# Fused attention and experts: two heads of a pair in row tiles of 64, and twenty bias blocks moved between the first expert matmuls

## The chip, the core and the metric
The kernel runs as one program on one core of a Trainium2 chip. The metric is the device time of one execution in microseconds; three runs of the kernel before gave 641.36, 644.32 and 647.19 us, median 644.32. All inputs and the output are float32 and lie in DRAM. PE is the matrix engine; DVE is VectorE, ACT is ScalarE, POOL is GpSimd, and SP is the engine whose queue issues nearly all transfers.

## The reference
```python
# attention: B, H, S, D = 2, 8, 576, 64
scores = D**-0.5 * q @ k.T
pos = arange(S)
rel = abs(pos[:, None] - pos[None, :])
x = log1p(rel) / log1p(maximum(pos[:, None], 1))
h = maximum(x[..., None] @ w1 + b1, 0)        # 32 hidden units
bias = h @ w2                                  # one value per head
scores = scores + bias.transpose(2, 0, 1)[None]   # the same for both batches
attn = exp(scores - max(scores, -1))
attn = attn / (sum(attn, -1) + 1e-9)
x = (attn @ v) as rows (B*S, H*D) = (1152, 512)
# experts: E, F = 4, 1024
p = domain_probs / (domain_probs.sum(-1) + 1e-9)
out = sum over e of p[:, e] * (maximum(x @ w1[e], 0) @ w2[e])
```
Every expert works on every row.

## The kernel before, in words
The engines run side by side, each with its own instruction stream, and meet at semaphores. The order of the work is written out by hand for each engine; there is no planner.

**Bias blocks.** The bias of all heads is made once, in 36 blocks of 16 query rows, and written to a DRAM scratch, from where it is read back in rows of 128. A block has four `hidden` tiles of 128 x 576: DVE makes three (L573), ACT one (L745), in a ring of three blocks. PE multiplies each with a weight block of 32 columns (L874), so that four such products fill one score bank (column tiles of 32; the trace records each of these matmuls twice). ACT scales the sums into one of four row buffers (L752), and SP stores them (L395). The two score banks alternate.

**Split into high and low parts.** Score and expert matmuls use the type float32r. A number is split in a rounded high part and the rest, and a product is made of three or four partial products. For q and k POOL does this per head ("unit"): q and k of one head, D = 64 rows, are loaded twice, onto both halves of the 128 partitions; `q_parts` holds q's high part on one half and its low part on the other, and so one matmul over 128 rows against `k_hi`, and one against `k_lo`, give all four partial products (L900). A block of 128 query rows takes four matmuls, two for each half of 288 key columns.

**Attention in two parts.** Rows 0 to 255 of each sequence come first (f = 0), the other 320 later (f = 1). There are 8 pairs of heads. A pair has four blocks of 128 rows in part 0 (two per head), and in part 1 four and a fifth that holds the last 64 rows of both heads. A block goes: score (PE, L900), bias added and maximum found (DVE, L590), exp and row sum (ACT, L770), reciprocal (DVE, L600 and L603), normalised (DVE in part 0, L610; POOL in part 1, L540), transposed (PE, L918 and L922, into the turn banks), copied (ACT L776, DVE L616). Then come the products with v (PE, L940: the two heads side by side as column tiles of 64), and x is split (ACT L782, DVE L622). In part 0 both score banks are used in turn, so the next block's scores are made while a block is read; in part 1 only bank 0 is, and the two halves of bank 1 belong to the experts.

**Experts.** The four experts run first on the 512 early rows (ge 0 to 3, each 16 positions: 8 hidden tiles and 4 output tiles in two halves), then on the other 640 (ge 4 to 7). Weights come in chunks of 512 KB; ACT makes the high part (L796), DVE the low part (L628). A hidden tile is 12 or 24 matmuls (L960), an output tile 24 (L977), in a ring of three banks (`M_RING`). Between the positions of ge 0 to 3 stand the "slots" of attention part 1, six for each pair, from position 0 on; 50 of the 64 positions have one.

`split_count`, `score`, `turn`, `products` and `slot` (PE), `add_bias`, `invert` and `normalise` (DVE), and `load_raw`, `load_bias0`, `load_bias1` and `store_rows` (SP) are the functions that the change rewrites.

Of the kernel before, what the change touches and what calls it, by code (L numbers as in the profile page):

```python
# [9 lines left out]
ALU = mybir.AluOpType  # L10
# [20 lines left out]

TABLE_W = 2 * S - G
# [5 lines left out]
ON_DVE = QUADS - 1  # L38

# [4 lines left out]
UNITS = 2 * PAIRS  # L44
# [3 lines left out]
Q_W = ROWS0 + 3 * D  # L48
TURNS = (5, 7)

# [4 lines left out]
SLOTS = 6  # L55
CHUNK = 1024
# [12 lines left out]
def kq_slot(u):  # L69
    return u % 5 if u < UNITS else (u - UNITS + 1) % 3  # L70


def last_block_of(u):

    f, p, side = u // UNITS, u % UNITS // 2, u % 2
    return blk(0, p, 2 * side + 1) if f == 0 else blk(1, p, 4)


def before_in_slot(u):

    return next((o for o in range(u - 1, -1, -1) if kq_slot(o) == kq_slot(u)), None)


ACT_TURNS = ((0, 1, 3), (0, 1, 2, 3, 4, 5, 6))
# [80 lines left out]
M_RING = 3  # L165


def attention_and_experts(nc, qk_t, v, b_w, probs_in, w1, w2,
# [3 lines left out]
    with ExitStack() as top:  # L172
# [13 lines left out]
        k_hi = sb(top, "k_hi", [P, 3, S], F32R)  # L186
        k_lo = sb(top, "k_lo", [P, 3, S], F32R)
        q_parts = sb(top, "q_parts", [P, 3, Q_W], F32R)
# [3 lines left out]
        probs_t = sb(top, "probs_t", [P, 2, JT, ROWS1])  # L192
        ident = sb(top, "ident", [P, P])
# [13 lines left out]
        with ExitStack() as early:  # L207
            hidden_sb = sb(early, "hidden", [P, HID_RING, QUADS, S])
            rows = sb(early, "rows", [P, ROW_RING, S])
            table = sb(early, "table", [P, TABLE_W])  # L210
            probs_2 = sb(early, "probs_2", [P, BLKS[0], S])
            bias_2 = sb(early, "bias_2", [P, BLKS[0], S])
            kx_hi = sb(early, "kx_hi", [P, 2, S], F32R)
            kx_lo = sb(early, "kx_lo", [P, 2, S], F32R)
            qx_parts = sb(early, "qx_parts", [P, 2, ROWS0], F32R)
# [8 lines left out]
        turn_bank = [top.enter_context(nc.psum_tensor(f"turn{r}", [P, 512], F32)) for r in range(2)]  # L224
# [12 lines left out]
        v_in = [sem(f"v_in{r}") for r in range(4)]  # L237
        bias0_in = [sem(f"bias0_in{r}") for r in range(2)]
        bias1_in = [sem(f"bias1_in{r}") for r in range(3)]
        qk_split, scored, maxed, exped = (sem(s) for s in ("qk_split", "scored", "maxed", "exped"))  # L240
        plus_eps, recip_done, normed0, normed1 = (
            sem(s) for s in ("plus_eps", "recip_done", "normed0", "normed1"))
# [7 lines left out]
        SMALL_DMAS, CLEARED = G + 1, 4  # L250


        def hidden(n, quad):
            return hidden_sb[:, n % HID_RING, quad, :]
# [5 lines left out]
        def k_of(u):  # L260
            s = kq_slot(u)
            return (k_hi[:, s, :], k_lo[:, s, :]) if s < 3 else (kx_hi[:, s - 3, :], kx_lo[:, s - 3, :])

        def q_of(u):
            s = kq_slot(u)
            return q_parts[:, s, :] if s < 3 else qx_parts[:, s - 3, :]

        def split_count(u):

            return 4 * (u + 1) if u < UNITS else 4 * UNITS + 6 * (u + 1 - UNITS)  # L270
# [7 lines left out]
        def score_of(n):  # L278
            return score_bank[n % 2 if n < BLKS[0] * PAIRS else 0]

        def m_bank(n):
            return (score_bank[1][:, 0, :], score_bank[1][:, 1, :], last_bank[:, :])[n % M_RING]

        def sub_in(f, n, i):
            bank = turn_bank[n % 2]
            if i < 4:
                return bank[:, :].rearrange("p (t q) -> p t q", t=4)
            if i == 4:
                return bank[0:J_LAST, :].rearrange("p (r q) -> p r q", r=2)
            if i == 5:  # L290
                return bank[:, :].rearrange("p (t r q) -> p t r q", t=4, r=2)
            return bank[0:J_LAST, 0:P].rearrange("p (r q) -> p r q", r=2)

        def sub_out(f, i):
            if i < 4:
                return probs_t[:, i // 2, 0:4, P * (i % 2):P * (i % 2) + P]
            if i == 4:
                return probs_t[0:J_LAST, :, 4, 0:ROWS0]
            if i == 5:
                return probs_t[:, :, 0:4, ROWS0:ROWS1].rearrange("p r t q -> p t r q")  # L300
            return probs_t[0:J_LAST, :, 4, ROWS0:ROWS1]

        def x_slice(x, f, p):
            m, b = p // 2, p % 2
            first = ROWS0 * b if f == 0 else TOK0 + ROWS1 * b
            return x[:, m, first:first + (ROWS0, ROWS1)[f]]
# [28 lines left out]

        def free_bank(eng, n):

            if n >= M_RING:
                kind, ge, i, c = BANK_ORDER[n - M_RING]
                if kind == "h":  # L340
                    eng.wait_ge(hidden_lo, h_taken_n(ge, i, c, c) + 1)
                else:
                    eng.wait_ge(y_out, y_n(ge, i) + 1)
            elif n < 2:
                eng.wait_ge(maxed, blk(0, PAIRS - 1, 3) + 1)

        with nc.Block() as block:

            @block.sync
            def _(sp):  # L350
                def load_raw(u):
                    if u >= 2:
                        sp.wait_ge(qk_split, split_count(u - 2))
                    p = u % UNITS // 2
                    src = qk_t[p % 2, 2 * (p // 2) + u % 2]
                    for part in (slice(0, D), slice(D, P)):
                        sp.dma_start(qk_raw[part, u % 2, :, :], src).then_inc(raw_in[u % 2], 16)

                def load_v(f, p):
                    n = PAIRS * f + p  # L360
                    if n >= 2:
                        sp.wait_ge(weighed, n - 1)
                    for side in range(2):
                        slot = (2 * n + side) % 4
                        src = v[p % 2, 2 * (p // 2) + side]
                        sp.dma_start(v_sb[:, slot, 0:4, :],
                                     src[0:4 * P, :].rearrange("(t p) d -> p t d", p=P)
                                     ).then_inc(v_in[slot], 16)
                        sp.dma_start(v_sb[0:J_LAST, slot, 4, :], src[4 * P:S, :]).then_inc(v_in[slot], 16)

                def load_bias0(m):
                    if m >= 2:
                        sp.wait_ge(maxed, blk(0, 2 * m - 3, 3) + 1)
                    to = bias_2 if m % 2 else bias
                    for side in range(2):
                        src = bias_dram[2 * m + side, 0:ROWS0, :].rearrange("(t p) j -> p t j", p=P)
                        sp.dma_start(to[:, 2 * side:2 * side + 2, :], src).then_inc(bias0_in[m % 2], 16)

                def load_bias1(m, part):

                    if m == 0:
                        sp.wait_ge(maxed, blk(0, 5, 3) + 1)
                    else:
                        sp.wait_ge(maxed, blk(1, 2 * m - 1, (1, 3, 4)[part]) + 1)
                    if part < 2:
                        src = bias_dram[2 * m + part, ROWS0:4 * P, :].rearrange("(t p) j -> p t j", p=P)
# [6 lines left out]
                def store_rows(n):  # L393
                    sp.wait_ge(scaled, n + 1)
                    sp.dma_start(bias_dram[:, n * BLOCK_Q:(n + 1) * BLOCK_Q, :].rearrange("h i j -> i h j"),  # L395
                                 rows[:, n % ROW_RING, :]).then_inc(rows_stored[n % ROW_RING], 16)

                def load_chunk(n):
# [8 lines left out]
                    else:  # L407
# [9 lines left out]
                sp.dma_start(ident[:, :], eye).then_inc(eye_in, 16)  # L417
                load_v(0, 0)
                load_v(0, 1)
                sp.dma_start(p_raw[:, 0:2, :], probs_in[0:ROWS0, :].rearrange("(t p) e -> p t e", p=P)  # L420
                             ).then_inc(p_in, 16)
                sp.dma_start(p_raw[:, 2:4, :], probs_in[S:S + ROWS0, :].rearrange("(t p) e -> p t e", p=P)
                             ).then_inc(p_in, 16)
# [657 lines left out]
```

## Time and profile before
| | |
|---|---|
| Median of 3 runs | 644.32 us (641.36 to 647.19) |
| The profiled execution, its own time | 643.48 us |
| Its span, first to last instruction | 641.7 us |
| Granted PE clock, mean | 0.979 of full speed |
| Busy: PE | 585.5 us (91%) |
| Busy: weight loads of PE | 474.0 us (74%) |
| Busy: DVE, ACT, POOL | 332.1, 265.3, 152.9 us |
| Moved by DMA | 82.13 MB, 128 GB/s in the mean |

Busy time is that in which an engine has an instruction under way, waits left out. Matmuls are pipelined: a record of one lasts longer than the distance to the next, so the pace is read from the starts. The granted clock says which share of PE's full speed (2.4 GHz) the chip allowed in a stretch; 0.5 is the lower level, 1.2 GHz. The share of 91% is a mean over stages that are limited by different engines.

### The profile page before, as it was taken

How to read it: one execution, taken by the hardware profiler on the slowest of the kernel's cores; microseconds unless marked ns; L12 is line 12 of the kernel's file. 1: busy time of each engine (PE TensorE's matmuls, PEld its weight loads, DVE VectorE, ACT ScalarE, POOL GpSimd, SP SyncE). 2: the span in 40 equal slices, each digit the busy share in tenths (PEclk: the TensorE clock that was granted, in tenths of full speed). 3: DMA queues.
4: the chain of work that ended last, by engine and by line, in shares of the span. 5: the costliest groups of instructions: out<-in, count | busy, mean ns of one | idle time of the engine just before them, and what ended most of it. 6: DMA issues, size and time to landing. Idle time of an engine off the chain costs nothing.

```text
span 641.7 us, 9432 instructions
## 1 busy us (share of the span) xinstructions
PE 585.5 (91%) x3592; PEld 474.0 (74%) x3592; DVE 332.1 (52%) x701; ACT 265.3 (41%) x506; POOL 152.9 (24%) x208
## 2 busy tenths in 40 slices
PE   3867788768699999999899999999999999999997
PEld 1322466556577787887777877899899889989986
DVE  6998798974553456424562444254236225324511
ACT  4786745562553455433653443044025105402400
POOL 5052485720344535526343100000000000000000
PEclk9798989898899999999999999999999999999999
DMA  7799778972656346724750223332114023311301
GB/s 160 199 279 344 211 197 170 222 199 84 164 163 165 89 122 173 213 56 127 223 153 1 65 84 115 114 115 99 50 49 137 29 65 99 100 65 34 99 34 49
DMA packets 63724, 82.13 MB, mean 128 GB/s; under 512 B 24256, under 2 KB 40896, under 8 KB 63680
## 3 DMA queue, kind: packets, MB, share of 16 engines
q1 hardware_dynamic: 63488, 81.52, 45.1%
q8 instruction: 29, 0.48, 0.3%
q14 instruction: 15, 0.12, 0.1%
q10 hardware_dynamic: 192, 0.01, 0.0%
HBM read 68.53 MB, written 12.98 MB: 127 GB/s over the span
## 4 chain that ended last, share of the span: by engine, by line
PE 72%; DVE 12%; ACT 6%; issue 5%; DMA 3%; SPq 0%; ACTq 0%; DVEq 0%
PE scores L960 19%; PE scores L977 17%; PE m_bank L977 14%; PE m_bank L960 7%; PE x_bank L940 6%; PE scores L900 4%; DVE probs L590 3%; PE turn L918 3%; DVE hidden L573 3%; DVE w_lo L628 3%; DMA bias_scratch<-rows 3%; ACT w_hi L796 2%; PE scores L874 2%; ACT probs L770 2%; ACT rows L752 1%
## 5 line engine op out<-in xcount | busy, mean ns | idle before, releaser
L628 DVE TENSOR_TENSOR w_lo<-w_raw,w_hi 128x1024 fp32r<-128x1024 f32 x64 | 82.8, 1294 | 49.6 <-ACT w_hi L796 49.4
L960 PE MATMUL scores<-x_hi,w_hi 128*128 128x512 f32 (+2 forms) x272 | 93.6, 344 | 5.6 <-DVE w_lo L628 5.6
L803 ACT ACTIVATE h_hi<-scores 128x512 fp32r<-128x512 f32 (+2 forms) x68 | 30.8, 453 | 161.2 <-PE scores L960 161.2
L960 PE MATMUL scores<-x_hi,w_lo 128*128 128x512 f32 (+2 forms) x272 | 91.7, 337 | 0.0
L960 PE MATMUL scores<-x_lo,w_hi 128*128 128x512 f32 (+2 forms) x272 | 91.5, 336 | 0.0
L770 ACT ACTIVATE probs<-probs,neg_max 128x576 f32<-128x576 f32 x72 | 56.0, 777 | 67.4 <-DVE neg_max L590 67.4
L590 DVE CUSTOM_DVE_ANT_0 probs<-scores,bias 128x576 f32<-128x576 f32 x72 | 54.0, 750 | 29.7 <-PE scores L900 29.6
L874 PE MATMUL scores<-hidden,w_block 128*32 128x288 f32 x576 | 47.4, 460 | 22.3 <-ACT hidden L745 8.8
L796 ACT CAST w_hi<-w_raw 128x1024 fp32r<-128x1024 f32 x64 | 66.5, 1046 | 0.4 <-DMA w_raw<-w_in 0.3
L540 POOL TENSOR_SCALAR probs<-probs,recip 128x576 f32<-128x576 f32 x40 | 30.0, 751 | 147.5 <-DVE recip L603 147.5
L776 ACT COPY probs_t<-turn 128x512 f32<-128x512 f32 (+2 forms) x80 | 41.6, 552 | 56.9 <-PE turn L918 56.8
L977 PE MATMUL scores<-w_hi,h_hi 128*128 128x512 f32 x160 | 63.4, 396 | 0.0
L977 PE MATMUL scores<-w_hi,h_lo 128*128 128x512 f32 x160 | 62.5, 391 | 0.0
L977 PE MATMUL scores<-w_lo,h_hi 128*128 128x512 f32 x160 | 62.3, 390 | 0.0
L960 PEld LDWEIGHTS scores<-x_hi,w_hi 128*128 128x128 f32 x272 | 51.5, 189 | 12.0 <-issue 8.8
L635 DVE SCALAR_TENSOR_TENSOR h_lo<-scores,h_hi 128x512 fp32r<-128x512 f32 (+2 forms) x68 | 34.6, 508 | 48.4 <-ACT h_hi L803 28.6
L573 DVE TENSOR_SCALAR hidden<-table,shift 128x576 f32<-128x576 f32 x108 | 56.1, 596 | 3.9 <-PE scores L874 3.8
L940 PE MATMUL x_bank<-probs_t,v 128*64 128x256 f32 (+1 forms) x320 | 46.6, 442 | 10.4 <-issue 8.0
L874 PEld LDWEIGHTS scores<-hidden,w_block 128*32 128x32 f32 x576 | 18.2, 119 | 51.0 <-ACT rows L752 26.4
L960 PEld LDWEIGHTS scores<-x_hi,w_lo 128*128 128x128 f32 x272 | 51.4, 189 | 4.1
L960 PEld LDWEIGHTS scores<-x_lo,w_hi 128*128 128x128 f32 x272 | 51.5, 189 | 3.3
L900 PE MATMUL scores<-k_hi,q_parts 128*128 128x288 f32 x136 | 39.9, 311 | 8.8 <-DVE neg_max L590 8.5
(80 smaller groups left out, 1076.6 us busy)
## 6 DMA issues: line engine op xcount, KB each, us to landing
w_raw<-w_in SPq DMA_DIRECT2D x64, 512.0 KB, 3.6
qk_raw<-qk_t_in SPq DMA_DIRECT2D x64, 288.0 KB, 4.4
bias_scratch<-rows SPq DMA_DIRECT2D x36, 288.0 KB, 4.1
bias<-bias_scratch SPq DMA_DIRECT2D x16, 576.0 KB, 6.1
v<-v_in SPq DMA_DIRECT2D x32, 128.0 KB, 3.7
out_dram<-acc SPq DMA_DIRECT2D x8, 256.0 KB, 2.0
bias<-bias_scratch SPq DMA_DIRECT2D x8, 144.0 KB, 4.3
table<-distance_in SPq DMA_DIRECT2D x1, 574.0 KB, 4.3
```

Source lines behind the costliest of these rows:

```text
L573: dve.tensor_scalar(hidden(n, quad), window(group), shift[:, group:group + 1], 0.0, ALU.add, ALU.max).then_inc(hid_dve, 1)
L590: dve.tensor_tensor_reduce(probs_of(f, p, j).rearrange("p (c j) -> p c j", c=2), score_of(n)[:, :, 0:HALF], bias_of(f, p, j).rearrange("p ...
L628: dve.tensor_tensor(lo, raw, hi.bitcast(F32), ALU.subtract).then_inc(w_lo_out, 1)
L635: dve.scalar_tensor_tensor(lo, bank[:, cols], 0.0, hi.bitcast(F32), ALU.max, ALU.subtract).then_inc(hidden_lo, 1)
L770: act.activation(tile, tile, ACT.Exp, scale=-1.0, bias=neg_max[:, n % 10:n % 10 + 1], accum_out=row_sum[:, n % 10:n % 10 + 1]).then_inc(ex ...
L776: act.copy(sub_out(f, i), sub_in(f, n, i)).then_inc(out_act, 1)
L796: act.copy(hi, raw).then_inc(w_hi_out, 1)
L874: mm = pe.matmul(score_bank[n % 2][C * quad:C * quad + C, c, 0:HALF], w2_block[:, :, :].rearrange("p g h -> p (g h)"), hidden(n, quad)[:, ...
L900: mm = pe.matmul(score_of(n)[:, c, 0:HALF], q_of(u)[:, first:first + P], k[:, cols], start=side == 0 and part == 0, stop=side == len(sides ...
L940: mm = pe.matmul(x_bank[D * side:D * side + D, 0:width], v_sb[:, (2 * n + side) % 4, t, :], probs_t[:, side, t, 0:width], start=t == 0, st ...
L960: mm = pe.matmul(m_bank(n)[:, 0:width], w, x, start=k == 0 and part == 0, stop=k == MT - 1 and part == 2)
L977: mm = pe.matmul(m_bank(n), h, w[:, ft, :], start=ft == 0 and part == 0, stop=ft == FT - 1 and part == 2)
```

## The change
Part 1, **a pair shares the partitions**. Head 0 of a pair now lies on partitions 0 to 63 and head 1 on 64 to 127, loaded by one transfer. POOL splits q and k once for both heads, into `q_hi`, `q_lo`, `k_hi` and `k_lo` (SPLITS: 4 steps a pair early, 8 late). A score step makes 128 query rows of both heads: three partial products (high-high, low-high, high-low) on each half of the key columns, each as two matmuls over 64 partitions, head 0 into score bank 0 and head 1 into bank 1, 12 matmuls in all. The block of the last 64 rows of both heads takes six full matmuls. Blocks are numbered so that j % 2 is the head.

Part 2, **order of attention part 0**. It goes in 16 steps of two blocks; the transposes follow two steps later (`LAG`). POOL normalises in part 0 as well, DVE makes the reciprocals of two blocks with one instruction each, a second `probs_t2` takes every other pair's transposed values, and the first weight chunk stands behind the copies in DVE's order.

Part 3, **bias blocks 16 to 35** (`EARLY` = 16) leave the first stage. Two of them stand at each of the positions 0 to 9 of ge 0; their buffers are parts of `probs`, `bias` and `probs_t`, and two hidden buffers stand where there were three. Early rows of the bias are read back in two parts, the second after block 15 is stored.

Part 4, **banks and slots**. Slots begin at position 12 (`FIRST_SLOT`), 50 of them as before. Part 1 of attention uses both score banks; the experts use three banks up to the third output tile of ge 0 and then two until the slots are over, and four after that. Products of part 1 go into free columns of score bank 0, in two halves of 160 columns.

```diff
+EARLY = 16
+LAG = 2
+FIRST_SLOT = 12
-M_RING = 3
+def bank_place(n):
+    if n < WOVEN_FROM:
+        return (3, 0, 1)[n % 3]
+    if n < WOVEN_END:
+        return 2 + n % 2
+    return n % 4
...
+        def sum_bank(n):
+            return score_bank[n % 2] if n < EARLY else (score_bank[0], turn_bank)[n % 2]
...
 # SP
-                    for part in (slice(0, D), slice(D, P)):
-                        sp.dma_start(qk_raw[part, u % 2, :, :], src).then_inc(raw_in[u % 2], 16)
+                    sp.dma_start(qk_raw[:, g % 2, :, :],
+                                 qk_t[p % 2, 2 * m:2 * m + 2].rearrange("h d a s -> (h d) a s")
+                                 ).then_inc(raw_in[g % 2], 16)
...
+                for n in range(1, EARLY):
                     store_rows(n)
...
+                rows_all_stored(EARLY)
+                load_bias0(0, 1)
+                load_bias0(1, 1)
...
+                        if ge == 0 and EARLY + 2 * pos < BLOCKS:
+                            store_rows(EARLY + 2 * pos)
+                            store_rows(EARLY + 2 * pos + 1)
...
+                        if ge == 0 and EARLY + 2 * pos == BLOCKS:
+                            rows_all_stored(BLOCKS)
+                            for part in range(3):
+                                load_bias1(0, part)
 # POOL
+                for s in range(STEPS + 1):
+                    if s >= 1:
+                        normalise(0, (s - 1) // 2, (s - 1) % 2)
+                    g = s // 2 + 2
+                    if 2 <= s and g < PAIRS + 2:
+                        if s % 2 == 0:
+                            high_of_qk(g)
+                        else:
+                            low_of_qk(g)
 # DVE
+                for s in range(STEPS + LAG + 1):
+                    p, t = s // 2, s % 2
+                    if s < STEPS:
+                        add_bias(0, p, 2 * t)
+                        add_bias(0, p, 2 * t + 1)
+                    if 1 <= s <= STEPS:
+                        invert(0, (s - 1) // 2, (s - 1) % 2)
+                    if LAG <= s < STEPS + LAG:
+                        take_turn(0, (s - LAG) // 2, 2 * (s % 2) + 1)
+                    if s >= LAG + 2 and t == 0:
+                        low_of_x(0, p - 2)
+                    if s == STEPS - 1:
+                        low_of_chunk(0)
+                    if s == STEPS:
+                        hidden_of_block(EARLY)
+                        low_of_chunk(1)
 # DVE, each position of ge 0 to 3
+                        if pos < FT:
+                            low_of_hidden(ge, pos)
+                        elif pos % 2:
+                            add_output(ge, (pos - FT) // 2)
                         n = chunk_at(ge, pos)
                         if n is not None:
                             low_of_chunk(CHUNK_N[n])
+                        if ge == 0 and EARLY + 2 * pos + 2 < BLOCKS:
+                            hidden_of_block(EARLY + 2 * pos + 2)
+                            hidden_of_block(EARLY + 2 * pos + 3)
+                        if 0 <= at < SLOTS * PAIRS + 2:
+                            slot(at)
 # ACT, the same places
+                        if ge == 0 and EARLY + 2 * pos < BLOCKS:
+                            scale_block(EARLY + 2 * pos)
+                            scale_block(EARLY + 2 * pos + 1)
+                        if ge == 0 and EARLY + 2 * pos + 2 < BLOCKS:
+                            hidden_of_block(EARLY + 2 * pos + 2)
+                            hidden_of_block(EARLY + 2 * pos + 3)
 # PE
+                def score_step(f, p, t):
...
+                        pe.wait_ge(maxed, blk(f, p, 2 * t) if f == 0 or t else blk(1, p, 0))
+                    if f == 1 and t == 1 and p >= 1:
+                        pe.wait_ge(x_lo_out, g)
+                    (kh, kl), (qh, ql) = k_of(g), q_of(g)
                     for c in range(2):
+                        for part, (q, k) in enumerate(((qh, kh), (ql, kh), (qh, kl))):
+                            for side in range(2):
+                                half = slice(D * side, D * side + D)
+                                mm = pe.matmul(score_bank[side][:, c, 0:HALF], q[half, P * t:P * t + P],
+                                               k[half, HALF * c:HALF * c + HALF],
+                                               start=part == 0, stop=part == 2)
+                    mm.then_inc(scored, 2)
...
+                for s in range(STEPS + 1):
+                    p, t = s // 2, s % 2
+                    if s < STEPS:
+                        score_step(0, p, t)
+                    if s >= LAG:
+                        turn(0, (s - LAG) // 2, 2 * (s % 2))
+                        turn(0, (s - LAG) // 2, 2 * (s % 2) + 1)
+                    if s >= LAG and t == 1:
+                        turn(0, p - 1, 4)
+                    if s >= LAG + 2 and t == 0:
+                        products(0, p - 2)
...
+                        if ge == 0 and EARLY + 2 * pos < BLOCKS:
+                            sum_block(EARLY + 2 * pos)
+                            sum_block(EARLY + 2 * pos + 1)
+                        if 0 <= at < SLOTS * PAIRS + 2:
+                            slot(at)
```

## Rows read from the trace of the kernel before
**Rows 1.** Busy time by stage: us, then busy and count per engine, clock, DMA.
```profile
8.78:69.64 60.86, 47.31 (x576) 18.17 (x576) 54.55 (x105) 46.30 (x70) 20.49 (x20) 0.92 0.86 251
69.64:151.51 81.87, 61.53 (x424) 48.08 (x421) 67.37 (x182) 42.84 (x96) 44.29 (x56) 0.92 0.73 182
151.51:416.38 264.87, 254.60 (x1352) 205.45 (x1350) 121.77 (x258) 114.83 (x211) 85.90 (x124) 0.99 0.45 126
416.38:641.70 225.32, 222.07 (x1249) 202.31 (x1247) 84.68 (x147) 58.20 (x126) 0.00 (x0) 1.00 0.23 74
```
**Rows 2.** Windows of line L874: us, PE busy, weight loads busy, clock, DMA.
```profile
36.25:69.64 33.39, 24.96 (x320) 9.41 (x320) 0.95 0.96 300
26.32:34.09 7.77, 7.07 (x96) 2.50 (x96) 1.00 0.91 267
```
**Rows 3.** Lines of DVE in 69.64:141.9: count, busy us, mean ns, idle before.
```profile
L590 DVE CUSTOM_DVE_ANT_0 probs<-scores,bias 128x576 f32<-128x576 f32 x32 | 23.9, 747 | 6.2 <-PE scores L900 6.2
L610 DVE TENSOR_SCALAR probs<-probs,recip 128x576 f32<-128x576 f32 x29 | 23.5, 810 | 1.0
L603 DVE RECIPROCAL recip<-recip 128x1 f32<-128x1 f32 x29 | 4.7, 164 | 1.0
L600 DVE TENSOR_SCALAR recip<-row_sum 128x1 f32<-128x1 f32 x30 | 4.3, 143 | 0.0
```
**Rows 4.** Timeline of PE at two products; waits of PE, whole span.
```profile
134.86 2.38 PE L940 MATMUL x_bank<-probs_t,v 128*64 128x256 f32 x20 [0.59 <-ACT probs_t L776]
...
146.07 3.70 PE L940 MATMUL x_bank<-probs_t,v 128*64 128x256 f32 x20 [5.01 <-issue]
...
PE scores L960 <- DVE w_lo L628: 5.6, 6, 2.0
```
**Rows 5.** Line group of POOL's normalising, whole span.
```profile
L540 POOL TENSOR_SCALAR probs<-probs,recip 128x576 f32<-128x576 f32 x40 | 30.0, 751 | 147.5 <-DVE recip L603 147.5
```
**Rows 6.** Timeline of PE: start us, us, instruction.
```profile
359.15 0.29 PE L900 MATMUL scores<-k_hi,q_parts 128*128 128x288 f32 x1
359.28 0.29 PE L900 MATMUL scores<-k_lo,q_parts 128*128 128x288 f32 x1
...
359.69 0.60 PE L918 MATMUL turn<-ident,probs 128*128 128x128 f32 x4
360.04 0.47 PE L977 MATMUL m_bank<-w_hi,h_hi 128*128 128x512 f32 x1
...
362.66 0.40 PE L977 MATMUL m_bank<-w_hi,h_lo 128*128 128x512 f32 x1
```
**Rows 7.** Timeline of weight loads, the first two of a block.
```profile
70.70 0.19 PEld L900 LDWEIGHTS scores<-k_hi,q_parts 128*128 128x128 f32 x1 [0.49 <-issue]
...
70.81 0.19 PEld L900 LDWEIGHTS scores<-k_lo,q_parts 128*128 128x128 f32 x1
```
**Rows 8.** Timeline of PE from scores to products.
```profile
349.50 0.29 PE L900 MATMUL scores<-k_lo,q_parts 128*128 128x288 f32 x1
349.73 2.91 PE L940 MATMUL x_bank<-probs_t,v 128*64 128x320 f32 x20
```
**Rows 9.** Line groups of DVE and ACT, whole span.
```profile
L628 DVE TENSOR_TENSOR w_lo<-w_raw,w_hi 128x1024 fp32r<-128x1024 f32 x64 | 82.8, 1294 | 49.6 <-ACT w_hi L796 49.4
...
L635 DVE SCALAR_TENSOR_TENSOR h_lo<-scores,h_hi 128x512 fp32r<-128x512 f32 x24 | 16.4, 684 | 21.2 <-ACT h_hi L803 21.2
...
L796 ACT CAST w_hi<-w_raw 128x1024 fp32r<-128x1024 f32 x64 | 66.5, 1046 | 0.4 <-DMA w_raw<-w_in 0.3
L745 ACT ACTIVATE hidden<-table,shift 128x576 f32<-128x576 f32 x36 | 27.6, 772 | 0.5 <-DVE table L563 0.5
L752 ACT ACTIVATE rows<-scores,row_scale 128x576 f32<-128x576 f32 x36 | 26.6, 740 | 14.8 <-PE scores L874 10.2 <-DMA bias_scratch<-rows 4.4
```
**Rows 10.** Transfers in 18:75: count, KB each, median us from issue to landing.
```profile
bias_scratch<-rows SPq DMA_DIRECT2D x33, 288.0 KB, 4.4
...
bias<-bias_scratch SPq DMA_DIRECT2D x4, 576.0 KB, 6.8
```

More of the change, by code:

```diff
@@ L66, in turn_n, with inverted, place_of, before_in_place @@
     return TURNS[0] * p + i if f == 0 else TURNS[0] * PAIRS + TURNS[1] * p + i
[L69 to L84, printed above, removed]
+def inverted(f, p, t):
+    return 2 * p + t + 1 if f == 0 else STEPS + 3 * p + t + 1
+def place_of(g):
+    return g % 3 if g < PAIRS else g % 2
+def before_in_place(g):
+    return next((o for o in range(g - 1, -1, -1) if place_of(o) == place_of(g)), None)
+def last_block_of(g):
+    f, p = g // PAIRS, g % PAIRS
+    return blk(f, p, BLKS[f] - 1)
+ACT_TURNS = ((0, 2, 4), (0, 1, 2, 3, 4, 5, 6))
 def turn_taken():
@@ L164, with bank_before @@
 BANK_N = {k: n for n, k in enumerate(BANK_ORDER)}
-M_RING = 3
+WOVEN_FROM, WOVEN_END = BANK_N["y", 0, 2, 0], BANK_N["h", E, 0, 0]
+def bank_place(n):
[4 more added lines that the diff above has]
+    return n % 4
+def bank_before(n):
+    return next((o for o in range(n - 1, -1, -1) if bank_place(o) == bank_place(n)), None)
 def attention_and_experts(nc, qk_t, v, b_w, probs_in, w1, w2,
@@ L395, in store_rows, with rows_all_stored @@
                     sp.dma_start(bias_dram[:, n * BLOCK_Q:(n + 1) * BLOCK_Q, :].rearrange("h i j -> i h j"),
-                                 rows[:, n % ROW_RING, :]).then_inc(rows_stored[n % ROW_RING], 16)
+                                 rows_of(n)).then_inc(rows_stored[n % ROW_RING], 16)
+                def rows_all_stored(blocks):
+                    for r in range(ROW_RING):
+                        sp.wait_ge(rows_stored[r], 16 * (blocks // ROW_RING))
                 def load_chunk(n):
@@ L574, in _ @@
                                           ALU.add, ALU.max).then_inc(hid_dve, 1)
+                for n in range(EARLY):
+                    hidden_of_block(n)
                 def add_bias(f, p, j):
@@ L760, in _ @@
                 hidden_of_block(1)
[L761 to L762 removed]
+                for n in range(EARLY):
+                    if n + 2 < EARLY:
                         hidden_of_block(n + 2)
@@ new lines, in score_last @@
+                def score_last(p):
+                    g = PAIRS + p
+                    pe.wait_ge(maxed, blk(1, p, 3))
+                    (kh, kl), (qh, ql) = k_of(g), q_of(g)
+                    for c in range(2):
+                        for part, (q, k) in enumerate(((qh, kh), (ql, kh), (qh, kl))):
+                            mm = pe.matmul(score_bank[0][:, c, 0:HALF], q[:, ROWS0:Q_W],
+                                           k[:, HALF * c:HALF * c + HALF],
+                                           start=part == 0, stop=part == 2)
```

613 lines of the change are left out of this document (296 added, 317 removed).

## The prediction
> **What bounds the kernel now.** I cut the execution at the stage borders first [rows 1]: the bias blocks (8.78 to 69.64), attention on the first query rows (to 151.51), attention on the rest between the matmuls of experts 0 to 3 (to 416.38), and four experts alone. In the last, PE is busy 222.07 of 225.32 us and nothing of the change touches it: 0. In the third PE is busy 254.60 of 264.87, so there whatever is added to PE is added to the time. In the first two it isn't PE: VectorE has 54.55 of 60.86 and 67.37 of 81.87. Next, the pace of the first stage [rows 2]: 96 PE records, six blocks, in 7.77 us, so 1.3 us a block at best, while the last twenty blocks took 33.39 us, 1.67 each. Third, VectorE's work there by line [rows 3]: 23.9 us add the bias, 23.5 normalise, 9.0 are reciprocals, on columns of one element. Stage two is VectorE's, and near its end PE also stood 5 us, because VectorE had queued a weight chunk ahead of a copy that the products wait for [rows 4].
>
> **Stage one: 20 blocks leave it.** Block 16 starts at 36.25, the last block ends at 69.64: -33.4 us. The first score waits for the last scale as now, 1.1 us, and so starts at about 37.3.
>
> **Stage two.** Normalising goes to GpSimd: VectorE's 67.4 lose 23.5, and with one reciprocal pair per two blocks 4.5 more [rows 3]; 39.4 are left, 4.9 a pair. GpSimd takes over 4 x 0.75 a pair [rows 5], and the shared split runs once a pair instead of twice: its 44.3 us [rows 1] become about 44.3 / 2 + 24 = 46, 5.8 a pair. ScalarE keeps its 42.8, 5.4 a pair. All three stay under what follows. What sets the pace next is the ring between PE and VectorE: a step's two heads now fill both score banks, so the next step's scores wait for both bias adds.
>
> The unknown is a step's cost on PE: 12 matmuls of 64 rows, two by two in row tiles. Today two blocks are 8 matmuls at 0.134, 1.07 us (359.15 to 359.28, and 359.69 after four) [rows 6]. No row here has row tiles. The nearest are these.
> - Column tiles do run side by side: 16 records of the bias block with 288 columns end within 1.3 us, which is 81 ns each, where a full-array record of the same 288 columns takes 134 [rows 2, 6].
> - Two weight loads in a row stand 0.11 us apart [rows 7], and one is spent on every matmul.
> - A change of array shape costs: the products start 0.23 after the last score matmul instead of 0.134 [rows 8]: 0.1 going in, and I take 0.1 coming out.
>
> This bounds the step from below at 6 x 0.134 + 0.1 for the first second-tile load + 0.2 = 1.1 us (loads of both tiles overlap), in the middle at 6 x 0.22 + 0.2 = 1.5 (matmuls overlap, loads queue), and above at 12 x (0.134 + 0.11) + 0.2 = 3.1 (every matmul waits for its own load). I take 1.1, since the nearest row, the column tiles, shows real overlap and keeps its loads hidden. The bias block's weights have 32 columns, though, and here there are 128; hence the other ends stay in the range. The Trainium skill pulls both ways here. "TensorEngine Tiling (Array Packing)", Key Properties, says that different tiles can load weights and multiply in parallel, and that changing the tiling mode drains the engine: by this page the step is near 1.1. "TensorE: Matmul & The Clock Gate", LDWEIGHTS (loading the stationary operand), says that a load's time follows its columns, not its rows, so half-height loads save nothing: if the two tiles share one load path this speaks against the change, and gives the 1.5. The 0.11 us agrees with its P / 1.2, 107 ns; neither page's claim on row tiles is shown by a run here.
>
> Steps of even number carry on PE 1.1 + 8 transposes of 0.11 (four stand in 0.35, from 359.69 to 360.04) [rows 6] + products 2.4 [rows 4], 4.4 us. Odd ones have only 12 transposes and are bound by the ring: scores 1.1, 0.2 until their last result, two adds of 0.75 [rows 3], 0.2 for the semaphores, 3.0 us. The first four steps have no products: 3.0 each. Six even and five odd steps follow: 27 + 15 = 42, and from the last scores to the first expert matmul 6 us (last transposes, products of pair 6, chunk 0: ScalarE 1.05, VectorE 1.3 [rows 9]; the copy is now ahead of the chunk, so the 5 us hole goes). One new wait: the bias of rows 128 to 255 can be read back only when blocks 8 to 15 are in DRAM. A store takes 4.4 us and a load 6.8 [rows 10], behind a queue already 0.86 busy [rows 1], so it lands near 47 where step 1 wants it at 41: +6 us, and PE, VectorE and ScalarE all stand behind it. Sum: 37.3 + 12 + 42 + 6 + 6, plus 3 for stretches at the low clock (0.92 granted in both early stages [rows 1]): the experts start at 106 instead of 151.5, **-45.5**.
>
> **Stage three.**
> - Twenty bias blocks come between 10 expert matmul groups. A group of 12 takes 2.85 us (360.04 to 362.66 and one more) [rows 6]. Two blocks add at most 2 x 1.25 (24.96 us busy for 20 [rows 2]), at least 2 x 1.0, and two shape changes. VectorE has per position 6 x 0.43 for hidden (three make a 1.3 us block [rows 2]), 0.68 and 1.29 for experts, about 4.9 with the wait for ScalarE; ScalarE 2 x 0.77, 2 x 0.74 and 1.05, 4.1, and the high half of a hidden tile [rows 9]. All three engines lie at 4.7 to 5.5. I take 5.3: 10 x (5.3 - 2.85) = +24.5. GpSimd and SP's stores (two a position, 4.4 us each, four buffers) are covered.
> - Scores: 16 steps of 1.1 and 8 last blocks of 6 x 0.134, against 192 x 0.134 now: 24.0 - 25.7 = -1.7.
> - Products in two halves of 160 columns, 40 records instead of 20: 0.2 a pair, +1.6.
> - The bias for rows 256 on is read back after block 35, 4.4 + 6.8 us, while PE has positions 10 to 13 (11 us) before it needs the result: 0 to 5, I take 1. Of today's stalls in this stage (264.87 less 254.60 is 10.3 us; 5.6 of them on w_lo [rows 4]) I let 5 go: -4 together.
> Sum **+20.4**.
>
> **Sum.** -45.5 + 20.4 = -25.1 on a span of 641.7, so 616.6; +3 for small waits of so new an order, +1.8 that lies around the span (643.48 against 641.7): 621. The profiled execution's 643.48 is 0.84 below the median 644.32; I compare with the latter.
>
> **Rivals.**
> - *Loads queue* (step 1.5): +0.4 x 32 = +13: 634. For it: the 0.11 between loads. Against: the column tiles. Chance 0.24; the first case has 0.50.
> - *Row tiles don't overlap*, so that the change isn't what it says: 12 x 0.134 + 0.2 = 1.8, +0.7 x 32 = +22: 643, no difference. Chance 0.12.
> - *The weave stalls*: with overlap, but each of the ten positions at 7 us since two hidden buffers tie PE, ScalarE and VectorE in one ring: +17, 638. For it: today's ring with three buffers makes 1.67 a block rather than 1.3. Chance 0.08.
> - *Slower*: each row-tile matmul waits for its own load, in score steps of both attention stages; step 3.1, +2.0 x 32 = +64, 685. It decides from a step of 2.05 us on (621 + 32 x 0.95 = 651). Against it: today matmuls of 0.29 us start every 0.134, each with its own load, so loads do overlap with running matmuls [rows 6]. Chance 0.06.
>
> About 1% (6.4 us) is what a measurement here can tell from no change. Faster: 0.5 and 7 in 10 of the 634 case, and parts of the two near 640: 0.69. Same: 0.19. Slower: 0.12, the last rival and unforeseen waits. The first case alone has 611 to 632 (weave 4.9 to 5.8, bias wait 3 to 10 us). To leave out no more than 2 in 10 the range takes in loads that queue and tiles that don't overlap: 609 to 648.
>
> **What would show it.** Score matmuls of 64 rows in couples whose starts are a few ns apart, couple to couple 0.134 (0.22: loads queue; single file at 0.134: no overlap). Experts starting at 106. A VectorE wait of about 6 us for bias at step 1. Positions of 5.3 us in the weave and 285 us for stage three, the last stage at 225.3. The forecast is wrong if the step is over 1.5, if stage two keeps 80 us, or if stage three grows by more than 33.

## The result, and the profile after

| | before | after |
|---|---|---|
| Median | 645.76 us (4 runs, 641.36 to 647.28) | 617.88 us (4 runs, 615.99 to 619.06) |
| Profiled execution: its own time, span | 643.48, 641.7 | 619.06, 617.2 |
| Ratio | | 0.9576 (95% interval 0.9519 to 0.9634) |
| Busy: PE, DVE, ACT, POOL | 585.5, 332.1, 265.3, 152.9 | 581.0, 296.1, 262.7, 119.7 |
| Moved by DMA | 82.13 MB | 72.72 MB |

The change makes the kernel 4.2% faster. PE has about as much to do as before (581.0 for 585.5 us); what shrank is above all the time in which it stood, 36.2 us instead of 56.2, which is 20.0 of the 24.5 us by which the span is shorter. The busy times by stage of the changed kernel answer to [rows 1]. Columns: stretch in us, its length, then busy us and count of PE, weight loads, DVE, ACT and POOL, the granted clock, DMA share, GB/s. The stages are bias blocks 0 to 15, attention part 0, part 1 between the experts, and experts alone.

```profile
9.39:43.26 33.87, 25.43 (x257) 9.50 (x258) 23.69 (x45) 20.49 (x31) 11.36 (x12) 0.88 0.70 207
43.26:108.46 65.20, 56.71 (x480) 40.57 (x480) 41.62 (x116) 39.72 (x93) 46.04 (x64) 0.90 0.55 164
108.46:391.94 283.48, 276.75 (x1883) 215.66 (x1881) 141.80 (x289) 141.12 (x253) 60.06 (x93) 0.99 0.43 129
391.94:617.20 225.26, 222.07 (x1249) 202.28 (x1247) 84.58 (x147) 58.21 (x126) 0.00 (x0) 1.00 0.23 73
```

Against [rows 1] the first score stands at 43.26 instead of 69.64 (-26.4), stage two takes 65.20 instead of 81.87 (-16.7), stage three 283.48 instead of 264.87 (+18.6), stage four the same. The sum is -24.5, the difference of the spans. In stage two DVE has 41.6 us of work where it had 67.4, and PE is busy for 0.87 of it instead of 0.75.

**A score step** at the full clock, in PE's timeline (start us, us, instruction); it answers to [rows 6, 8]:

```profile
100.82 0.40 PE L1000 MATMUL scores<-k_hi,q_hi 64*128 64x288 f32 x2
101.05 0.30 PE L1000 MATMUL scores<-k_hi,q_lo 64*128 64x288 f32 x2
101.19 0.29 PE L1000 MATMUL scores<-k_lo,q_hi 64*128 64x288 f32 x2
101.32 0.29 PE L1000 MATMUL scores<-k_hi,q_hi 64*128 64x288 f32 x2
101.45 0.29 PE L1000 MATMUL scores<-k_hi,q_lo 64*128 64x288 f32 x2
101.59 0.29 PE L1000 MATMUL scores<-k_lo,q_hi 64*128 64x288 f32 x2
101.81 1.19 PE L1029 MATMUL turn<-ident,probs 128*128 128x128 f32 x8
```

Each line is a couple (x2), the two heads at once with starts 3 to 4 ns apart, and the couples stand 0.133 apart, the pace of single full-array matmuls before. The first has 0.23 to the second, and the transposes start 0.22 after the last: 101.81 - 100.82 is 1.0. The first matmul also starts later after another array shape: 0.32 us after the start of an expert matmul, where the full-row scores of an experiment below stand 0.23 behind one. With this 0.09 the step is 1.08.

**The weave.** First the stretch of positions 0 to 2, whose expert matmuls PE had done before 121.26 and whose six blocks now catch up, with the expert group of position 3; then six steady positions. The columns are as above:

```profile
121.26:136.64 15.38, 11.11 (x109) 5.89 (x108) 12.83 (x24) 11.38 (x17) 0.00 (x0) 0.89 0.74 203
136.64:166.76 30.12, 30.12 (x265) 18.68 (x264) 22.69 (x44) 22.35 (x32) 0.00 (x0) 1.00 0.61 183
```

The steady part is PE's alone, 30.12 of 30.12 us, 5.02 a position: 12 expert matmuls in 2.94 and two blocks of 1.00 and 1.08. The first stretch isn't: PE stands 4.3 us and the clock is at 0.89. In the second trace of the same kernel, where no low clock fell into it, the stretch took 13.8 us instead of 15.4.

**The start of stage two** comes late, and its first steps are slow. SP's timeline, around the first read-back of bias:

```profile
25.67 2.57 SPq L458 DMA_DIRECT2D bias_scratch<-rows  x3
32.84 0.38 SPq L441 DMA_DIRECT2D bias<-bias_scratch  x1
```

DVE's timeline, the bias add of step 1:

```profile
50.59 0.76 DVE L699 CUSTOM_DVE_ANT_0 probs<-scores,bias 128x576 f32<-128x576 f32 x1 [3.92 <-DMA bias<-bias_scratch]
```

Busy times from the start of stage one to the experts (columns as in the stages):

```profile
9.39:28.00 18.61, 16.15 (x164) 6.20 (x168) 18.20 (x33) 12.50 (x20) 7.58 (x8) 1.00 0.58 137
28.00:32.84 4.84, 2.11 (x32) 0.68 (x24) 4.12 (x10) 2.44 (x5) 1.51 (x2) 0.91 0.72 266
32.84:43.26 10.42, 7.17 (x65) 2.63 (x66) 1.38 (x3) 5.54 (x8) 2.28 (x3) 0.66 0.89 303
43.26:50.59 7.33, 3.61 (x24) 2.95 (x24) 1.45 (x5) 1.62 (x4) 0.00 (x0) 0.50 0.65 215
50.59:56.00 5.41, 3.82 (x22) 3.25 (x24) 3.46 (x13) 2.56 (x6) 1.52 (x3) 0.51 0.42 167
56.00:108.46 52.46, 49.28 (x436) 34.38 (x436) 36.72 (x100) 35.53 (x84) 44.52 (x62) 1.00 0.55 157
```

Between 28.24 and 32.84 SP issues nothing: it waits until the first eight blocks are stored, so that it may read their bias back, and the finished rows of later blocks queue behind it. PE is busy 2.11 of 4.84 us there; the clock granted is 0.91 in that stretch, 0.66 in the next and 0.50 then, and only from 56 on is it full again. That the hole in the stores brought the low clock isn't shown by this trace alone. DVE's 3.92 is the wait for the second part of the bias.

Waits of PE and ACT over the whole span (waited for: us in total, times, longest):

```profile
PE scores L1000 <- DVE neg_max L699: 5.3, 2, 3.6
PE turn L1029 <- POOL probs L627: 3.3, 4, 1.0
...
ACT rows L845 <- DMA bias_scratch<-rows: 6.8, 4, 2.4
```

So GpSimd, which now normalises everything, hardly holds PE up: 3.3 us in all.

### The profile page after: what moved, and what is told of

Its sections match the earlier page's. It is cut to its first block, busy times and chain, and to the rows that moved or that the text cites. A ratio compares the mean times of both kernels' runs of the same rounds, so it can differ in the third digit from the quotient of the medians.

```text
span 617.2 us, 9758 instructions
## 1 busy us (share of the span) xinstructions
PE 581.0 (94%) x3864; PEld 468.1 (76%) x3864; DVE 296.1 (48%) x608; ACT 262.7 (43%) x506; POOL 119.7 (19%) x176
## 2 busy tenths in 40 slices
DMA packets 60654, 72.72 MB, mean 118 GB/s; under 512 B 23232, under 2 KB 39872, under 8 KB 60608
## 4 chain that ended last, share of the span: by engine, by line
PE 84%; DMA 4%; ACT 4%; DVE 3%; issue 2%; POOL 2%; SPq 0%; ACTq 0%; DVEq 0%; POOLq 0%
PE m_bank L1095 12%; PE scores L1078 11%; PE x_bank L1095 11%; PE m_bank L1078 10%; PE scores L1095 10%; PE x_bank L1078 9%; PE turn L1029 5%; PE scores L1000 4%; PE scores L1058 4%; PE scores L968 3%; DMA bias_scratch<-rows 3%; PE x_bank L1058 3%; PE turn L968 2%; PE turn L1033 1%; DVE hidden L679 1%
## 5 line engine op out<-in xcount | busy, mean ns | idle before, releaser
L1029 PE MATMUL turn<-ident,probs 128*128 128x128 f32 x288 | 45.2, 285 | 3.4 <-POOL probs L627 3.3
L1078 PE MATMUL scores<-x_hi,w_hi 128*128 128x384 f32 (+2 forms) x148 | 47.8, 323 | 0.0
L1078 PE MATMUL scores<-x_lo,w_hi 128*128 128x384 f32 (+2 forms) x148 | 47.3, 319 | 0.0
L1078 PE MATMUL scores<-x_hi,w_lo 128*128 128x384 f32 (+2 forms) x148 | 47.2, 319 | 0.0
L1078 PE MATMUL m_bank<-x_hi,w_hi 128*128 128x512 f32 (+2 forms) x124 | 44.9, 362 | 0.0
L1078 PE MATMUL m_bank<-x_hi,w_lo 128*128 128x512 f32 (+2 forms) x124 | 43.4, 350 | 0.0
L1078 PE MATMUL m_bank<-x_lo,w_hi 128*128 128x512 f32 (+2 forms) x124 | 43.4, 350 | 0.0
L1078 PE MATMUL x_bank<-x_hi,w_hi 128*128 128x512 f32 (+2 forms) x112 | 39.7, 354 | 0.0
L1095 PE MATMUL m_bank<-w_hi,h_hi 128*128 128x512 f32 x96 | 38.7, 403 | 0.0
L1078 PE MATMUL x_bank<-x_lo,w_hi 128*128 128x512 f32 (+2 forms) x112 | 38.5, 344 | 0.0
```

The source lines that it names most:

```text
L1029: mm = pe.transpose(bank[:, P * t:P * t + P], probs_of(f, p, j)[:, P * t:P * t + P], ident[:, :])
L1078: mm = pe.matmul(m_bank(n)[:, 0:width], w, x, start=k == 0 and part == 0, stop=k == MT - 1 and part == 2)
L1095: mm = pe.matmul(m_bank(n), h, w[:, ft, :], start=ft == 0 and part == 0, stop=ft == FT - 1 and part == 2)
```

## The experiments

Each was timed beside runs of the kernel before on its chip, whose medians were 643.27 to 644.47 us. All ratios are to the kernel before. Differences like +9.6 are to the median of the changed kernel in the run that comes next, 618.28 us; across chips they are good to about 1 us.

**The changed kernel again**, the base for the others.

> The changed kernel as it is, beside which the three others are read: 616 to 620 us again, 0.954 to 0.963 of the kernel before. No theory separates here.

Measured: 618.28 us (615.92 to 619.76), ratio 0.9609 (0.9551 to 0.9668). First score at 43.68, first expert matmul at 109.48, stage four from 391.34; these marks are the base below. It is what was expected.

**Heads one after the other.** Is it the alternation that lets the tiles overlap?

```diff
-for c in range(2):
-    for part, (q, k) in enumerate(...):
-        for side in range(2):
+for side in range(2):
+    for c in range(2):
+        for part, (q, k) in enumerate(...):
```

> Same 12 matmuls of 64 rows in a score step, but first the six of head 0 and then the six of head 1, so that neighbours share a row tile. Theory, the time rests on two row tiles running side by side: single file at 0.134 us, 12 x 0.134 against 0.77 + 0.14, so a step is 0.7 us longer, 32 steps, +22 us: about 640. Rival, the couples are not what pays (the gain is VectorE's relief and the moved blocks, and odd steps wait for VectorE anyway): under +6, so 618 to 624. Second rival, PE reorders or overlaps across the six: no change at all, and the starts in the trace still 0.07 apart.

Measured: 627.92 us (626.96 to 629.14), ratio 0.9766 (0.9719 to 0.9812): +9.6, between the 22 of the theory and the under 6 of the first rival. PE's timeline shows why, and that the second rival, overlap across the six, is half right:

```profile
65.96 0.40 PE L1000 MATMUL scores<-kx_hi,qx_hi 64*128 64x288 f32 x1
66.20 0.29 PE L1000 MATMUL scores<-kx_hi,qx_lo 64*128 64x288 f32 x1
66.33 0.29 PE L1000 MATMUL scores<-kx_lo,qx_hi 64*128 64x288 f32 x1
66.33 0.41 PE L1000 MATMUL scores<-kx_hi,qx_hi 64*128 64x288 f32 x2
66.57 0.31 PE L1000 MATMUL scores<-kx_hi,qx_lo 64*128 64x288 f32 x2
66.71 0.31 PE L1000 MATMUL scores<-kx_lo,qx_hi 64*128 64x288 f32 x2
66.84 0.29 PE L1000 MATMUL scores<-kx_hi,qx_hi 64*128 64x288 f32 x1
66.97 0.29 PE L1000 MATMUL scores<-kx_hi,qx_lo 64*128 64x288 f32 x1
67.11 0.29 PE L1000 MATMUL scores<-kx_lo,qx_hi 64*128 64x288 f32 x1
```

Three matmuls of head 0 go alone, then come three couples, then three of head 1 alone. Two matmuls on one tile stand 0.13 apart or more, and so the one that starts 7 ns after head 0's third can only be head 1's first, the seventh of the stream: it didn't wait for head 0's fourth to sixth, which start 0.12 us and more behind it. (A record doesn't name its head; this is read from the distances.) The first to last start is 1.14 us instead of 0.77, and 0.37 x 32 steps is 12, near the 9.6. So alternation isn't what makes the tiles overlap, but the order in which the matmuls are written decides how much of the overlap is had.

**Each score matmul over all 128 rows.** The count and the columns stay, the overlap goes; the scores are then sums over both heads.

```diff
-half = slice(D * side, D * side + D)
+half = slice(0, P)
```

> The 12 score matmuls of a step take all 128 rows instead of 64, so there are no row tiles and no change of array shape (the scores of the two heads are summed into both, which changes the output; the number of columns, banks and instructions stays). Theory: 12 x 0.132 = 1.6 us a step against 0.09 + 0.77 + 0.22 = 1.08, 32 steps on PE or on the ring of score banks: +16 us, 632 to 636. Rival, couples don't pay: under +5. The run with the heads one after the other can't decide it, since its trace shows that PE let head 1 start 0.37 us after head 0 and overlapped them still.

Measured: 631.36 us (629.76 to 633.23), ratio 0.9816 (0.9768 to 0.9864): +13.1, just below the 632 to 636 of the theory and far from the rival's under 5. A step of part 1, in PE's timeline:

```profile
208.17 0.42 PE L1000 MATMUL scores<-k_hi,q_hi 128*128 128x288 f32 x2
208.43 0.43 PE L1000 MATMUL scores<-k_hi,q_lo 128*128 128x288 f32 x2
...
209.48 0.43 PE L1000 MATMUL scores<-k_lo,q_hi 128*128 128x288 f32 x2
209.75 0.60 PE L1029 MATMUL turn<-ident,probs 128*128 128x128 f32 x4
```

Two now take 0.262, where a couple of row tiles takes 0.133; the step is 12 x 0.132 = 1.58 us, without a shape change. Stage three is 289.30 instead of 281.86 us (+7.4; 16 steps x 0.50 is 8), and the experts start 7.3 later. The two heads therefore do run at once on PE, and this is worth 13 us, net of the two changes of shape. It is what the layout would have lost without overlap; the prediction put that rival at 22, with the changes of shape left in.

**No weave**: all 36 bias blocks first, as before (EARLY = 36; the second part of the bias is read back after blocks 18 and 20 are issued).

```diff
-EARLY = 16
+EARLY = 36
...
```

> All 36 bias blocks in the first stage again, everything else as changed (slots still begin at position 12, bias of rows 128 to 255 is read back after block 18). Theory, the moved blocks earn little: the first stage grows by about 33 us less the wait for bias and the slow clock at the start of stage two (6 us), and stage three shrinks by what the blocks cost there, 121.26 to 168.84 less seven expert groups of 2.94, 27 us: 614 to 622. Rival, moving the blocks is the main gain: 626 or more.

Measured: 622.64 us (622.35 to 624.26), ratio 0.9688 (0.9642 to 0.9733): +4.4, at the upper edge of the theory (614 to 622) and well under the rival's 626. Moving the blocks isn't the main gain. The experts start 23.9 later, at 133.37, and stage three is 19.6 shorter. The start of that stage without bias blocks, as a window, and PE's longest wait for a chunk:

```profile
133.37:167.20 33.83, 28.27 (x130) 21.50 (x129) 16.37 (x27) 12.58 (x18) 3.16 (x5) 0.95 0.55 180
```
```profile
PE scores L1085 <- DVE w_lo L733: 4.4, 1, 4.4
```

PE stands 5.6 us of 33.8 there, mostly for the low part of a weight chunk. With the weave, twenty blocks at 1.04 us and 4.1 us of waits for them are 24.9, and the stage is only 19.6 longer; the 5.6 us hole that the blocks fill makes up the rest. This is worked out from the two traces, and wasn't tried by itself.

**Normalising back on VectorE in part 0**, all else as changed.

```diff
 # POOL, per step s
-if s >= 1:
-    normalise(0, (s - 1) // 2, (s - 1) % 2)
 # DVE, behind the reciprocals
+for j in range(2 * ((s - 1) % 2), 2 * ((s - 1) % 2) + 2):
+    dve.tensor_scalar(tile, tile, recip[...], None, ALU.mult)
```

> Normalising of part 0 is back on VectorE, behind the reciprocals; all else as changed. Theory, VectorE's relief is what lets PE set the pace of stage two: VectorE has 41.6 us in the stage and gets 32 x 0.52 to 0.81 more, its odd steps become 3.6 to 4.0 instead of 3.0 and the even ones 4.0 to 4.4: +5 to +11 us, 623 to 629. Rival, PE and the ring of score banks set the pace alone: under +2. Second rival, VectorE's order makes the ring pay all of it: +17 to +24, near 640.

Measured: 633.39 us (632.64 to 635.91), ratio 0.9857 (0.9807 to 0.9906): +15.1, above the 5 to 11 that I held likely and under the 17 to 24 of the second rival. The window from 43 to 122 us, and PE's longest wait in it:

```profile
43.00:122.00 79.00, 58.21 (x480) 42.68 (x480) 61.42 (x150) 40.08 (x94) 26.18 (x36) 0.88 0.47 143
```
```profile
PE turn L1032 <- DVE probs_t L717: 13.0, 7, 2.8
```

DVE is busy 61.4 of 79.0 us, so the length isn't its work alone: stage two is 13.0 us longer than in the base (78.8 for 65.8), and PE waits 13.0 us for DVE's copies of transposed values, a wait that the base doesn't have. The copies now stand behind normalising in DVE's queue and hold the turn banks. DVE is in the ring even with a fifth of its time idle.

**The same edit on the kernel before**: part-0 normalising to POOL, between its splits of single heads.

```diff
 # POOL
-for u in range(UNITS + 2):
-    split_qk(u)
+for p in range(PAIRS):        # five splits ahead
+    normalise0(p, 0); normalise0(p, 1); split_qk(2 * p + 5)
+    normalise0(p, 2); normalise0(p, 3); split_qk(2 * p + 6)
...
 # DVE, behind the reciprocal
-dve.tensor_scalar(tile, tile, recip[...], None, ALU.mult)
```

> The kernel before with one thing of the change: part 0 is normalised on GpSimd, between its splits; order, scores and blocks as before. Theory, stage two was VectorE's: its 67.4 us lose 23.5, and the stage falls from 82 us to what GpSimd (44.3 + 24 = 68) and PE (61.5) allow, 70 to 76, so 631 to 637. Rival, the relief is worth nothing without the new order in steps, since GpSimd now has to split two heads a pair as well and PE waits for each block: 641 to 647.

Measured: 648.16 us (643.08 to 650.49), ratio 1.0056 (1.0022 to 1.009): nothing gained, and just above the 641 to 647 of the rival. Stage two as a window, PE's waits in it, and the longest of them in the timelines of SP and PE:

```profile
69.60:154.40 84.80, 58.75 (x417) 45.07 (x416) 43.53 (x150) 43.29 (x96) 65.38 (x88) 0.92 0.69 173
```
```profile
PE x_bank L952 <- DMA v<-v_in: 11.0, 3, 6.4
PE turn L930 <- POOL probs L549: 7.1, 4, 2.8
```
```profile
97.14 1.11 SPq L357 DMA_DIRECT2D qk_raw<-qk_t_in  x2
98.30 0.59 SPq L366 DMA_DIRECT2D v<-v_in  x1
...
107.61 4.47 PE L952 MATMUL x_bank<-probs_t,v 128*64 128x256 f32 x20 [6.43 <-DMA v<-v_in]
```

DVE falls to 43.5 us, as after the change, and stage two is 84.8 long instead of 81.9. POOL has 65.4 us of work, and its splits come later. SP issues the load of raw q and k at 97.14, because it waits for a split, and the loads of v stand behind it: issued from 98.30 on, landed at 107.36. In the kernel before the same loads of v were issued from 93.32 on and had landed at 102.98, ahead of the products at 105.61. Such waits for v make 11.0 us of PE's time, those for normalised values 7.1. So in this place and with this order of loads the relief of VectorE isn't worth anything, while in the changed kernel it is worth 15. Whether loads of v ahead of those of q and k would have saved it wasn't tried; that the shared split makes the difference is read from POOL's work (65.4 for 46.0 us) and not shown by itself.

**Loads moved in the first stage**: the first read-back of bias goes behind block 11 instead of 8, and two loads behind the stage.

```diff
-if n == 8:
+if n == 11:
     rows_all_stored(EARLY // 2)
     load_bias0(0, 0)
-if n == 10:
-    load_raw(3)
-if n == 12:
-    load_bias0(1, 0)
 rows_all_stored(EARLY)
 load_bias0(0, 1)
+load_raw(3)
+load_bias0(1, 0)
 load_bias0(1, 1)
```

> Early reads of the bias and one load of q and k are moved in SP's order: the first bias read stands behind block 11 instead of 8, so that the stores of blocks 9 and 10 no longer queue behind its wait, and the third q and k load and the read for pairs 2 and 3 stand behind the reads that step 1 waits for. Theory, the first stage is held up by the SP queue and the transfers in it (ScalarE waited 6.8 us for row stores in the changed kernel, 2.4 of it at 29.6 behind SP's 4.6 us hole): first scores at 39 to 41 instead of 43.3, 3 to 5 us less, 613 to 615. Rival, the stage is VectorE's and GpSimd's (blocks 0 to 4 at 1.9 to 3.3 us) and the transfers only fill gaps: under 1 us, 617 to 619.

Measured: 614.46 us (613.25 to 615.25), ratio 0.9549 (0.9509 to 0.9589): -3.8 against the changed kernel, as the theory said. First stage as a window, and two waits over the whole span:

```profile
9.30:37.80 28.50, 22.09 (x252) 8.09 (x245) 23.79 (x44) 19.59 (x29) 10.99 (x12) 1.00 0.68 192
```
```profile
DVE probs L697 <- DMA bias<-bias_scratch: 9.7, 2, 5.4
ACT rows L843 <- DMA bias_scratch<-rows: 2.3, 1, 2.3
```

The first score is at 37.8, 5.9 earlier, at full clock throughout, and the wait for bias has grown from 3.8 in the base to 9.7, which takes part of it back. ScalarE's wait for row stores has shrunk from 7.9 to 2.3 us. So what SP did in the stage cost it its 6 us; the edit moves both the wait ahead of the stores and two loads out of the stage, and doesn't tell how much is due to each.

**Weight chunks behind the bias blocks** at positions 0 and 1, on ACT and DVE; and both edits together.

```diff
-if n is not None:
+behind = ge == 0 and pos < 2
+if n is not None and not behind:
     high_of_chunk(CHUNK_N[n])
...
+if behind:
+    high_of_chunk(CHUNK_N[n])
```

> At positions 0 and 1 the weight chunk is split behind the hidden tiles of the next bias blocks, on ScalarE and VectorE. Theory, in the first three positions of the weave, which have no expert matmuls left, PE waits for hidden tiles that stand behind the chunk (4 us of PE waits from 121.26 to 136.64): 1 to 3 us less, 615 to 617. Rival, the chunks are then late for the output tiles or for the chunk loads behind them: 0 or +1.

> Both changes of order together. If each takes away its own wait the gains add, 5 us in the middle: 611 to 615. If only one theory holds, that one's number.

Measured: 618.14 us (617.44 to 619.37), ratio 0.9611 (0.9574 to 0.9648), alone, and 614.98 us (612.99 to 615.87), ratio 0.9558 (0.9516 to 0.9599), with the loads moved: no change (-0.1), and nothing on top of the loads (614.98 for 614.46). The fourth weave position starts 14.1 us after the first, in the base 13.8, and PE's waits for hidden and scaled blocks in the weave are 4.4 us for 4.1: the chunks weren't what those blocks waited for.

**Twenty blocks first**, with the loads moved, so that the second read-back no longer waits for the last block.

```diff
-EARLY = 16
+EARLY = 20
...
-rows_all_stored(EARLY // 2)
+rows_all_stored(8)
...
-rows_all_stored(EARLY)
+rows_all_stored(16)
```

> The kernel with the later loads, with 20 blocks in the first stage instead of 16 (16 in the weave). Theory, PE, VectorE and ScalarE stand 5 us at step 1 because the bias of rows 128 to 255 waits for block 15's store and its own read, 9 us after the last scale; four blocks more cover it: the first stage +5.2, the wait -5, the weave -4 x 1.1: 609 to 613. Rival, what the wait costs is already used otherwise (slow clock and row stores follow the last block wherever it stands): 614 to 617.

Measured: 613.41 us (611.46 to 614.42), ratio 0.9527 (0.9489 to 0.9564), the lowest of all, yet only 1.0 below the version with 16, within the spread of both, and between the 609 to 613 of the theory and the 614 to 617 of the rival. The first score comes at 45.20 instead of 37.82 (+7.4, and not 5.2); the wait for bias falls from 9.7 to 3.4, but stage two gets only 1.8 us shorter, and the stages behind it 5.7. It is below the changed kernel by about 5 us; that it is faster than the version with 16 blocks isn't shown.

## Why the prediction was right

It said 621 us, range 609 to 648, by overlap of the row tiles; 617.9 came, and the mechanism is the one forecast. That it came so close to 621 owes something to errors that cancel, as the terms show.

- **The step on PE.** Taken at 1.1, measured 1.08. The nearest row, the column tiles, was the right guide, though not by the figure taken from it. The 81 ns against 134 compare unlike things: each column-tile matmul has two records, so a matmul takes 163 ns, and its operands are plain float32 and not float32r. What shows the overlap is that four records at a time start 7 ns apart (28.909 to 28.929 in the kernel before) and the next four come 0.24 us later, where full-array matmuls in a row stand 0.134 apart. Loads that queue (1.5) fall by the couples at 0.133, and "no overlap" by the full-row experiment, 1.58 and +13.1. By the Trainium skill, "TensorEngine Tiling (Array Packing)", Key Properties, different tiles load and multiply in parallel, and the trace agrees: the weight loads of a couple stand in one line of two, 3 ns apart by their starts, where two full-height ones stood 0.11 apart [rows 7]. Timeline of weight loads after the change:

```profile
63.41 0.19 PEld L1000 LDWEIGHTS scores<-kx_hi,qx_lo 64*128 64x128 f32 x2
```

- **But PE gained nothing by it.** Two blocks were 8 matmuls in 1.07 and are 12 in 1.08. Row tiles pay for the third partial product per head that the shared layout needs; the gain is what the layout allows: one split for both heads, and so room on GpSimd for normalising. The pair of experiments on normalising fits this: taking it back costs 15.1, giving it to the kernel before wins nothing, though there late loads of v took part of what it might have won. How much is due to the order of steps and how much to the shared split wasn't tried apart.
- **Stage one.** Forecast first score 37.3, measured 43.3: the term mis-sized most. I took the pace of the last twenty blocks for a constant and priced the new read-back only where it is used. Its wait also stands in SP's queue ahead of stores. With that wait and two loads moved it is 37.8.
- **Stage two.** Forecast 68.7 from the first score to the experts (106 less 37.3; the terms 12, 42, 6, 6 and 3 add to 69), measured 65.2. The eleven distances between steps 4 and 15 take 42.0 us for the 42 forecast, a pair 7.50 for 7.4 (the 42 was rounded up from 6 x 4.4 + 5 x 3.0 = 41.4). The first four steps take 15.5 for 21: the wait for bias is 3.9 and not 6, since the stage began 6.0 us later and the bias landed at 50.57, 3.6 later than forecast, and the low clock, there for 13 us of the stage (0.50 and 0.51 up to 56.0), lay largely under waits. From the last scores to the experts it is 7.6, forecast 6.
- **VectorE in stage two** has 41.6 us and not 39.4. The reciprocals of two blocks together saved about 2.5 us, not 4.5: over the stage they take 7.2 instead of 9.8. The first of the two instructions mostly lasts 0.16 us, but seven of the sixteen start while GpSimd is making a low part of k or q, last 0.37 to 0.69 us, and end 24 to 29 ns after GpSimd's instruction. That it is GpSimd that holds them up wasn't tried. Timelines of DVE and POOL:

```profile
68.84 0.41 DVE L711 TENSOR_SCALAR recip<-row_sum 128x2 f32<-128x2 f32 x1
67.80 1.42 POOL L613 TENSOR_TENSOR k_lo<-qk_raw,k_hi 128x576 fp32r<-128x576 f32 x1
```

- **Stage three.** Forecast 285, measured 283.5. The weave took 27 instead of 24.5: steady positions are 5.02 (5.3 forecast), and the first three lost 4.3 us of waits and, in this trace, 1.6 to the low clock. Products in halves of 160 columns cost 0.03 a pair, not 0.2. Stalls fell from 10.3 to 6.7 us.
- **Bias blocks moved as a whole**: my terms give -33.4 + 24.5 + 6 = -2.9; the experiment without the weave gives -4.4.
- **Stage four and around the span**: 0 forecast, 0 measured; 1.86 around the span for 1.8. The 3 us kept for small waits weren't needed on top of the 6 lost in stage one.

The errors (+6.0, -3.5, -1.8, and -3 not needed) had both signs; they sum to -2.3 on the span, 619.6 forecast with the 3 us and 617.2 measured. That the sum is this small is luck; the step on PE, the pair of steps and the last stage are not.

## What to carry to other kernels

Row tiles with half the contraction ran here in couples at the pace of one full matmul, when the two tiles alternated in the stream; they win time on PE only if the number of matmuls doesn't grow with them, as it did here from 8 to 12. Moving work off the busiest engine pays if the engine that takes it, and the queue that feeds that one, have an even place for it: ask who waits behind it, as with SP's loads of v. A wait for data to be stored and read back belongs behind the stores that other engines are short of.

## What the runs showed of the hardware

- Matmuls on one row tile start while matmuls ahead of them in the stream wait for the other tile: with the heads in turn, the seventh of the stream started 0.37 us after the first and 7 ns after the third (which is which is read from the distances).
- Weight loads of two row tiles overlap too, 3 ns apart, each 0.19 us long.
- A change of shape costs 0.09 us going into row tiles (0.32 from an expert matmul to a score matmul, 0.23 with full rows) and 0.09 coming out (0.22 from the last score matmul to a transpose, 0.133 with full rows).
- A TENSOR_SCALAR of VectorE on 128 x 2 elements mostly took 0.16 us, but 0.37 to 0.69 the seven times that it started under a TENSOR_TENSOR of GpSimd; it then ended 24 to 29 ns after GpSimd's. No experiment took the two apart.
- The granted clock was at the lower level, 1.2 GHz, for the first 13 us of stage two (0.50 and 0.51), after PE had been busy 2.11 of 4.84 us and then 7.17 of 10.42. With the loads moved stage one stayed at 1.00; the changed kernel had 0.88 there.
